# The second layer's products taken in pairs of passes: two narrow, two turns, then two wide without a break

## The reference

```python
def _moe2_ref(x, w_gate, w_output_gate, w1, w2):      # x: 3072 tokens x 512, 8 experts, F = 1024
    logits = x @ w_gate
    e_idx = np.argmax(logits, axis=1)
    gate_w = probs[np.arange(N), e_idx]
    eom = 1.0 / (1.0 + np.exp(-(x @ w_output_gate)))
    for e in range(E):
        mask = e_idx == e
        h = np.maximum(x[mask] @ w1[e], 0.0)
        out[mask] = gate_w[mask, None] * eom[mask, e, None] * (h @ w2[e])
```

## Time and profile before

| | |
|---|---|
| three runs | 502.85, 503.69, 507.48 us; median 503.69 us |
| profiled execution | 510.57 us, of which its span is 508.7 us |
| TensorE busy | 460.1 us, 90% of the span |
| ScalarE busy | 273.5 us, 54% |
| VectorE busy | 214.3 us, 42% |
| GpSimd busy | 185.0 us, 36% |
| granted TensorE clock, mean | 0.982 |

### The profile page before, as it was taken

The page is one execution under the profiler, slowest core; times in us unless marked ns, Lnnn a source line. Parts: engine busy times, 40 slices in busy tenths (PEclk is TensorE's granted clock), DMA queues, the critical chain, the costliest instruction groups (busy, mean ns, idle before and its releaser), DMA issues.

```text
span 508.7 us, 12976 instructions
## 1 busy us (share of the span) xinstructions
PE 460.1 (90%) x4601; PEld 252.1 (50%) x4602; DVE 214.3 (42%) x890; ACT 273.5 (54%) x464; POOL 185.0 (36%) x147
## 2 busy tenths in 40 slices
PE   2798999999998799896799999999999999999992
PEld 2687777777776543363543434343434343434330
DVE  1678988988988461038421212121212121212110
ACT  1466876776775410103225666565656565666540
POOL 2568877877877210002301222222222222222110
PEclk9999999999999999998969999999999999999998
DMA  9879999999999987999999775101010101010000
GB/s 149 152 238 194 254 276 183 275 272 172 273 278 229 381 263 268 422 428 429 406 383 403 295 289 188 45 22 44 23 44 22 44 22 44 23 44 22 22 2 0
DMA packets 98651, 95.66 MB, mean 188 GB/s; under 512 B 86680, under 2 KB 87128, under 8 KB 95928
## 3 DMA queue, kind: packets, MB, share of 16 engines
q1 hardware_dynamic: 94328, 73.38, 51.9%
q10 hardware_dynamic: 1008, 14.68, 7.4%
q0 software_dynamic: 3280, 7.15, 4.0%
HBM read 88.51 MB, written 7.73 MB: 189 GB/s over the span
## 4 chain that ended last, share of the span: by engine, by line
PE 60%; DMA 14%; SPq 11%; POOL 6%; issue 5%; ACT 2%; DVE 1%; POOLq 0%; ACTq 0%; DVEq 0%
PE bank L897 39%; DMA arena<-in_moe_w_dram 11%; PE bank L874 6%; POOL arena L541 3%; POOL arena L536 3%; SPq L406 3%; PE bank L675 2%; SPq L396 2%; DMA arena<-in_mem_v_dram 2%; PE bank L607 2%; SPq L408 2%; SPq L399 2%; PE bank L819 1%; PE bank L863 1%; PE bank L622 1%
## 5 line engine op out<-in xcount | busy, mean ns | idle before, releaser
L897 PE MATMUL bank<-arena 128*64 (+1 forms) x448 | 205.8, 604 | 0.0
L907 PE MATMUL bank<-arena 128*64 128x512 f32 x448 | 205.8, 604 | 0.0
L897 PEld LDWEIGHTS bank<-arena 128*64 128x64 f32 x448 | 57.5, 138 | 104.3 <-issue 99.3
L575 POOL DMA_INDIRECT out_dram<-arena,tok_sorted x28 | 28.4, 1013 | 194.4 <-ACT arena L1307 194.4
L1152 DVE TENSOR_SCALAR arena<-bank 128x256 f32<-128x256 f32 x112 | 39.7, 418 | 104.5 <-PE bank L874 104.5
L536 POOL TENSOR_TENSOR arena<-arena,row_inv 96x1024 f32<-96x1024 f32 x32 | 60.6, 1893 | 32.3 <-DVE row_inv L974 32.3
L541 POOL TENSOR_TENSOR arena<-arena,row_max 96x1024 f32<-96x1024 f32 x32 | 60.6, 1893 | 12.7 <-DVE row_max L981 12.7
L981 DVE CUSTOM_DVE_ANT_0 arena<-bank,masks 96x128 f32<-96x128 f32 x256 | 55.0, 277 | 9.7 <-PE bank L607 9.7
L907 PEld LDWEIGHTS bank<-arena 128*64 128x64 f32 x448 | 57.5, 138 | 0.0
L1332 ACT COPY arena<-arena 128x2048 f32 x27 | 51.2, 1898 | 9.3 <-issue 9.3
L1327 ACT COPY arena<-arena 128x2048 f32 x27 | 51.3, 1900 | 1.6 <-issue 1.3
(11 more groups left out here) (180 smaller groups left out, 577.0 us busy)
## 6 DMA issues: line engine op xcount, KB each, us to landing
arena<-in_moe_w_dram SPq DMA_DIRECT2D x18, 2048.0 KB, 10.2
arena<-in_moe_w_dram ACTq DMA_DIRECT2D x7, 2048.0 KB, 9.5
arena<-in_moe_w_dram SPq DMA_DIRECT2D x24, 512.0 KB, 8.3
arena<-in_v_dram SPq DMA_DIRECT2D x32, 240.0 KB
arena<-in_q_dram SPq DMA_DIRECT2D x32, 192.0 KB, 4.6
arena<-in_k_dram SPq DMA_DIRECT2D x20, 192.0 KB, 4.1
arena<-in_moe_w_dram SPq DMA_DIRECT2D x2, 1024.0 KB, 8.4
arena<-in_k_dram SPq DMA_DIRECT2D x4, 240.0 KB
```

What stands on the lines that cost most here:

```text
L897: mm(bank[4 + par][0:HR, :], h_t[:, par, lo:lo + HR], w2_all[:, bass.ds(at_w2 * SEG + f * DM, DM)], start=(f == 0), stop=(f == KF - 1))
L907: ins = mm(bank[4 + par][HR:TR, :], h_t[:, par, lo + HR:lo + TR], w, start=(f == 0), stop=(f == KF - 1))
```

## The change

The passes 0 to 4 (SINGLE = 5) keep their order, except that the register load stands behind the narrow products, and that pass 4 has the turns of 6 and 7 both in its middle. From then on, 11 pairs i = 3 to 13 are issued: narrow 2i, narrow 2i + 1, turn 2i + 2, turn 2i + 3, then the 8 wide steps of pass 2i - 1 and the 8 of pass 2i. The last pair has no turns, and the wide steps of pass 27 follow it. So a narrow product runs up to a pass and a half ahead of its wide one. To hold two passes at once, `c_t` and bank 6 are double, the narrow results of odd passes go to the second 256 columns of the banks 0 to 3, `c_rep` moves to another tile (`token_side`), and the ring of gathered rows has 8 places, of which 7 are filled ahead (LEAD = 7). VectorE and ScalarE are put into the pairs' order, and two of their waits are now for both passes of a pair.

```diff
-    CR = 4
+    CR = 8
-    ONE_BY_ONE = 6
+    SINGLE = 5
+    LEAD = 7
...
-            for j in range(CR):
+            for j in range(LEAD):
                 gather(j)
             for j in range(NP):
                 store(j)
-                if j + CR < NP:
-                    gather(j + CR)
+                if j + LEAD < NP:
+                    gather(j + LEAD)
...
-            with pe.Fori(ONE_BY_ONE // 2, (NP - 2) // 2) as i:
-                for par in range(2):
-                    step2(i * 2 + par, par, True, True, True)
-            for j in range(NP - 2, NP):
-                step2(j, j % 2, True, j + 1 < NP, False)
+            def pair(i, last):
+
+                layer1(2 * i, 0, True)
+                layer1(2 * i + 1, 1, False)
+                if not last:
+                    turn(2 * i + 2, 0, True)
+                    turn(2 * i + 3, 1, False)
+                layer2(2 * i - 1, 1, True)
+                layer2(2 * i, 0, True)
+
+            assert SINGLE % 2 == 1 and NP % 2 == 0
+            with pe.Fori((SINGLE + 1) // 2, NP // 2 - 1) as i:
+                pair(i, False)
+            pair(NP // 2 - 1, True)
+            layer2(NP - 1, 1, True)
...
             def relu2(j):
-                dve.wait_ge(l1_made, j + 1)
+                dve.wait_ge(l1_made, j + 1 if j <= SINGLE else j // 2 * 2 + 2)
                 if j >= 2:
                     dve.wait_ge(l2_made, j - 1)
...
+            for j in range(SINGLE + 1, NP, 2):
+                relu2(j)
+                relu2(j + 1)
+                if j + 4 < NP:
+                    spread(j + 4)
+                    spread(j + 5)
...
             def ct_copy(j):
 
-                if j >= 1:
-                    act.wait_ge(l1_made, j)
-                act.wait_ge(c_turned, j + 1)
-                sc.copy(c_t[:], bank[6][:, 0:TR]).then_inc(ct_copied, 1)
+                if j >= 2:
+                    act.wait_ge(l1_made, j - 1)
+                act.wait_ge(c_turned, j + 1 if j <= SINGLE else j // 2 * 2 + 2)
+                sc.copy(c_t[:, j % 2], bank[6][:, j % 2 * TR:(j % 2 + 1) * TR]).then_inc(ct_copied, 1)
...
+            for i in range((SINGLE + 1) // 2, NP // 2):
+                fill_high(2 * i)
+                if 2 * i + 2 < NP:
+                    ct_copy(2 * i + 2)
+                    ct_copy(2 * i + 3)
+                    pick(2 * i + 2)
+                    pick(2 * i + 3)
+                evacuate(2 * i - 1)
+                fill_low(2 * i + 1)
+                fill_high(2 * i + 1)
+                evacuate(2 * i)
+                if 2 * i + 2 < NP:
+                    fill_low(2 * i + 2)
+            evacuate(NP - 1)
```

More of the change, by code:

```diff
@@ L872, in layer1, with layer2 @@
                         for r in range(4):
-                            at = (2 * a + cc) * HR
+                            at = par * 2 * TR + (2 * a + cc) * HR
                             ins = mm(bank[r][:, at:at + HR], g_sel[par][32 * r:32 * r + NS, a, cc * 128:(cc + 1) * 128],
-                                     c_t[32 * r:32 * r + NS, a * HR:(a + 1) * HR], start=True, stop=True)
+                                     c_t[32 * r:32 * r + NS, par, a * HR:(a + 1) * HR], start=True, stop=True)
                 ins.then_inc(l1_made, 1)
-            def step2(j, par, more, do_l1, do_turn, inside=None, first=False):
+            def layer2(j, par, more, first=False, inside=()):
                 if first:
@@ L891, in step2 @@
                     if f == KF // 2:
[L892 to L895, removed]
+                        for kind, k in inside:
+                            if kind == "hidden":
+                                hidden(k)
+                            else:
+                                turn(k, k % 2, k <= SINGLE + 1)
                     lo = f * 128
@@ L914, in _ @@
             pe.wait_ge(g_copied, EARLY_G + 1)
-            for j in range(ONE_BY_ONE):
-                step2(j, j % 2, j >= 2, True, True, EARLY_G + 1 + j if EARLY_G + 1 + j < E else None, first=(j == 0))
-            with pe.Fori(ONE_BY_ONE // 2, (NP - 2) // 2) as i:
-                for par in range(2):
-                    step2(i * 2 + par, par, True, True, True)
-            for j in range(NP - 2, NP):
-                step2(j, j % 2, True, j + 1 < NP, False)
+            for j in range(SINGLE):
+                layer1(j + 1, (j + 1) % 2, True)
+                inside = [("hidden", EARLY_G + 1 + j)] if EARLY_G + 1 + j < E else []
+                inside += [("turn", j + 2)] + ([("turn", j + 3)] if j == SINGLE - 1 else [])
+                layer2(j, j % 2, j >= 2, first=(j == 0), inside=inside)
+            def pair(i, last):
[11 more added lines that the diff above has]
+            layer2(NP - 1, 1, True)
         @block.vector
@@ L1165, in _ @@
             relu2(0)
[L1166 to L1170, removed]
+            for j in range(SINGLE):
+                spread(j + 2)
+                if j == SINGLE - 1:
+                    spread(j + 3)
+                relu2(j + 1)
+            spread(SINGLE + 3)
+            spread(SINGLE + 4)
+            for j in range(SINGLE + 1, NP, 2):
+                relu2(j)
+                relu2(j + 1)
+                if j + 4 < NP:
+                    spread(j + 4)
+                    spread(j + 5)
         @block.scalar
@@ L1340, in _ @@
             fill_low(1)
-            for j in range(NP):
+            for j in range(SINGLE):
                 if EARLY_G + 1 + j < E:
                     g_copy(EARLY_G + 1 + j)
[L1344 to L1348, removed]
-                evacuate(j)
-                if j + 2 < NP:
-                    fill_low(j + 2)
+                pick(j + 2)
+                if j == SINGLE - 1:
+                    pick(j + 3)
+                ct_copy(j + 2)
+                if j == SINGLE - 1:
+                    ct_copy(j + 3)
+                fill_high(j + 1)
+                evacuate(j)
+                fill_low(j + 2)
+            for i in range((SINGLE + 1) // 2, NP // 2):
[12 more added lines that the diff above has]
+            evacuate(NP - 1)
 _INS = ["q", "k", "v", "mem_k", "mem_v", "moe_phi", "moe_w1", "moe_w2",
```

12 lines of the change are left out of this document (5 added, 7 removed).

## The result

The changed kernel has a median of 501.74 us over 12 runs; the kernel before, run beside it, 506.9 us over 12. The ratio is 0.9914, with a 95% interval of 0.9886 to 0.9941: 0.9% faster, 4.4 us by the ratio and 5.2 between the medians. (All ratios here compare executions in the chip's usual state; a few that ran in a slower one are left out.) Forecast were 495.1 us and 8.6 us saved; the kernel before, at 503.69 us when the forecast was made, has a median 3.2 us higher here, so the saving is what the forecast is held against. Two later measurements of the same kernel, each beside the kernel before, gave 1.0031 (1.0002 to 1.0060) and 1.0010 (0.9980 to 1.0041): no gain at all. Both findings have to be explained, a gain of half the size and its loss at other times.

A forecast was written before the change was run, and what follows sets the result against it. TensorE's own stream was taken as the bound. Pairs of 16.16 us against 16.96 save 0.80 in ten pairs, 0.74 in the last, less 0.11 in pass 4: 503.69 - 8.6 = 495.1 us, range 493.0 to 502.0.

The forecast's parts named there:

- What bounds the kernel: In the passes only TensorE's own stream counts: busy 204.00 of 204.00 us, with the clock full.
- Rival C: Evacuation, fill or pick ends later than TensorE needs it; ScalarE 1 us late would cost 11 us, 506; chance 0.06.
- Pieces 1 to 4: In a pair: narrow to narrow 0.89 us, narrow to turn 1.05, turn to turn 0.11, seam between wide blocks free.
- Rival A: In a pair's narrow blocks and turns, changing over and supply eat gain: 3.4 us saved in all, 500.3; chance 0.20.
- three changes of shape: In TensorE's stream a pair has three where two passes had eight, each costing 0.10 to 0.16 us.
- The register load: TensorE's load right before the wide products, taken at 0 within bounds of 0 and 0.97 us per pair.
- Rival B: Register load exposed, 0.97 us at 11 pairs and 4 single passes: 14.6 us, 509.7; chance 0.12, full or half.
- The three more gathers: At the start, about 4 us more GpSimd work before a first store that waits anyway; taken at 0.

The follow-up runs named there:

- after_again: The changed kernel as it is, measured once more on one chip with a repeat of load_first: ratio 1.0031 to the kernel before.
- split_turns: The changed kernel with a pair's first turn moved between its two narrow blocks: one execution, 2.77 us from first narrow block to the wide, no ratio given.
- load_first: The changed kernel with each pair's first register load ahead of its narrow blocks, likewise in passes 1 to 4: ratio 0.9896 to the kernel before, 0.9949 when repeated.
- written_out: The changed kernel with its ten pairs with turns written out instead of looped: one execution, first turn to first wide 0.37 us, period 16.20 us, no ratio given.
- ring_alone: The kernel before with only the ring of eight, seven gathers ahead and the tiles moved for it: ratio 1.0096.
- best: load_first with passes 3 and 4 also a pair, two gathers ahead of the one-hot products and five held back behind them: ratio 0.9875.
- ramp: The changed kernel with four gathers ahead, then two behind each of the first three stores: ratio 0.9902.
- ramp_best: load_first with passes 3 and 4 also a pair, and the gathers issued as in ramp: ratio 0.9807.
- before_load_late: The kernel before with only the register load put behind the narrow block, right before its wide products: ratio 1.0117.

## Why the prediction was wrong

**What bounds the kernel** held: only TensorE's own stream counts in the passes. Of all traces one has a wait for ScalarE there, of 0.2 us (after_again), and none for VectorE. Rival C fell. One reading was wrong: the clock is not full in the whole second half of the span, the slice from 254 to 267 us has a 6 in the earlier trace rows. The first wide products run in it, and the saving was reckoned as if the clock were full there; between the two profiled executions this makes 0.2 us.

**Pieces 1 to 4** held. Narrow to narrow 0.95 for 0.89, narrow to turn 1.00 for 1.05, turns 0.11 apart, and the seam between wide blocks costs nothing; with the load out of the way the stretch is 2.31 us, as summed, and the period 16.20 for 16.16, 0.4 us over ten pairs. Rival A fell. The sentence that the pair keeps three changes of shape at 0.10 to 0.16 us was right, by split_turns.

**The register load** is the first step that failed, taken at 0 within bounds of 0 and 0.97. It measured 0.28 us in each of the ten pairs with turns, 0.19 in the last pair (1.20 from its second narrow block to the wide, 1.01 in load_first) and 0.20 to 0.31 in four single passes: 10 x 0.28 + 0.19 + 4 x 0.24 = 4.0 us. This is Rival B at 4.0 of its 14.6 us. The reason given for 0, that the sequencer arrives with a long lead and has 1.4 us of narrow block and turns to hide in, left out what the loop adds in the same place (written_out), and that behind one narrow block, or two without turns, the load shows even where no loop is. That a narrow block uses up the lead twice as fast as it looks, with 32 loads of weights beside its 32 products in 0.9 us, may be why; it was not tried.

**The three more gathers** are the second step that failed, at other times than in the first measurement's trace: they were placed "between its last early gather and a first store that waits for the first evacuation anyway", and "All these I take at 0". I had asked who waits for GpSimd, and the answer, nobody, was right. I had not asked what GpSimd's work does to an engine that does not wait for it. In nine of the ten traces in which seven gathers meet the one-hot products it costs 3.7 to 4.8 us between the block's start and the first wide product, held against the kernel before, and 1% by ring_alone. The forecast's 8.6, less 4.0 for the load and 0.4 for the period, are the 4.1 to 4.3 us that the passes show, and less another 4 to 5 they are the 1.001 and 1.003 of two of the three measurements. In the profiled execution that was shown first the hold-up was absent. Of the 4.2 us by which it was ahead at the first wide product, 2.5 arise between the start of the block and that product; the other 1.7 are what is left, when the block begins, of an attention part that ended 3.9 us sooner, in code that is the same in both.

**The range**, 493.0 to 502.0 us, holds the measured 501.74 only just. Its high end was said to take in half of B, which by the prediction's own sum is 502.4. The gain that was measured is made of the forecast's pieces and a quarter of Rival B, a mixture that no line of the prediction had.

## What to carry to other kernels

Removing breaks from a saturated TensorE stream paid what the rows say, 0.76 us a pair (16.96 to 16.20) once the load was out of the way. It did so only where nothing that the sequencer does alone (a register load, a wait against a register, a loop's own work) stood between short instructions and the long ones that need it; issue such loads behind long instructions. When a ring is made deeper, fill it over the first rounds and not all at once: here gathers issued in a row went together with delays of engines that don't wait for them. And read one stage's length from the trace, since the spans of two executions agreed here with a wrong forecast to a tenth of a microsecond.

## What the runs showed of the hardware that was not expected

- GpSimd issuing indirect gathers back to back (1.25 us each) goes together with TensorE's products coming in pieces, 7.4 to 8.4 us for a block that takes 2.35 undisturbed, and with its signals being late: in best the end of a block at 254.04 was seen by two engines at 258. Of the ten traces with seven gathers in a row nine show it, and the five with four gathers show 2.4 to 4.2 us (2.35 in ramp, 2.97 in ramp_best). Why it is absent in one is open, and also by which way it acts (the supply with instructions, the signals, or TensorE itself); that was not tried. Seven plain loads did not show it.
- A load of a register on TensorE is free behind wide products (and load_first) and costs 0.29 us behind one narrow block, 32 products and their 32 weight loads (before_load_late). Behind two narrow blocks and two turns it costs 0.28 in the loop (the changed kernel) and nothing written out (written_out).
- A change of shape in TensorE's stream costs about 0.16 us (split_turns against load_first, two more changes for 0.31), where two narrow blocks behind each other start 0.95 us apart and two turns 0.11 (the changed kernel: two turns last 0.44 us and one 0.33).
